# The last tile of each sequence leaves out its state update in an fp32 linear-attention and two-FFN kernel

## The reference

```
state = zeros(B, H, D, D)
for t in range(S):                       # B=4, H=8, S=768, D=48
    kt, vt, rt = k[:, :, t], v[:, :, t], r[:, :, t]
    cur = einsum('bhd,bhe->bhde', u[None] * kt, vt)
    y[:, :, t] = einsum('bhd,bhde->bhe', rt, state + cur)
    state = w[None, :, :, None] * state + einsum('bhd,bhe->bhde', kt, vt)
```

## Time and profile before

| | us |
|---|---|
| Median of 3 executions | 806.8 |
| The three executions | 805.24, 806.8, 806.94 |
| The profiled execution, its own time | 806.01 |
| Its span, from the first to the last instruction | 804.3 |
| PE busy in the span | 739.9 (92%) |
| DVE busy | 425.6 (53%) |
| ACT busy | 304.3 (38%) |
| POOL busy | 149.6 (19%) |

### The profile page before, as it was taken

The page is one execution under the profiler, slowest core; times in us unless marked ns, Lnnn a source line. Parts: engine busy times, 40 slices in busy tenths (PEclk is TensorE's granted clock), DMA queues, the critical chain, the costliest instruction groups (busy, mean ns, idle before and its releaser), DMA issues. The chain is left out here.

```text
span 804.3 us, 12788 instructions
## 1 busy us (share of the span) xinstructions
PE 739.9 (92%) x4978; PEld 619.3 (77%) x4979; DVE 425.6 (53%) x677; ACT 304.3 (38%) x505; POOL 149.6 (19%) x170
## 2 busy tenths in 40 slices
PE   3789898999999999999999999999359999999995
PEld 2668687788877887788878888888249999998985
DVE  6778765575647565475746564544354323223232
ACT  2546443543445343544444443644233212122120
POOL 7433531222222211122222200000060000000000
PEclk9999988999999999999999999999769999999998
DMA  8792110211121111111110000000360202202021
GB/s 150 197 226 48 20 30 11 70 30 21 30 69 31 31 30 22 59 30 31 28 43 1 1 1 30 11 1 1 106 212 1 79 0 79 79 1 78 0 78 39
DMA packets 88316, 40.36 MB, mean 50 GB/s; under 512 B 77112, under 2 KB 84928, under 8 KB 88256
## 3 DMA queue, kind: packets, MB, share of 16 engines
q1 hardware_dynamic: 86800, 34.61, 17.2%
q10 hardware_dynamic: 1456, 4.93, 1.6%
HBM read 30.10 MB, written 9.44 MB: 49 GB/s over the span
## 5 line engine op out<-in xcount | busy, mean ns | idle before, releaser
L856 PE MATMUL x_ps<-g_p,wout_hi 128*128 128x512 f32 x576 | 186.7, 405 | 3.5 <-DVE g_p L672 3.4
L870 PE MATMUL h_ps<-x0T,win_hi 128*128 128x512 f32 x576 | 180.1, 394 | 1.2 <-DVE x0T L601 1.2
L472 ACT ACTIVATE above<-h_ps,minus_one 128x512 f32<-128x512 f32 x96 | 65.9, 687 | 196.4 <-DVE mid L681 196.4
L681 DVE TENSOR_SCALAR mid<-h_ps 128x512 f32<-128x512 f32 x96 | 66.2, 690 | 124.7 <-PE h_ps L870 124.5
L856 PEld LDWEIGHTS x_ps<-g_p,wout_hi 128*128 128x128 f32 x576 | 104.4, 190 | 32.3 <-DVE g_p L672 6.5
L870 PEld LDWEIGHTS h_ps<-x0T,win_hi 128*128 128x128 f32 x576 | 107.5, 189 | 24.4 <-DVE x0T L601 1.5
L1401 PE MATMUL ch_ps<-x_p,w_p 128*128 128x512 f32 x432 | 109.2, 400 | 11.9 <-DVE w_p L1467 11.9
L685 DVE TENSOR_TENSOR mid<-mid,above 128x512 f32<-128x512 f32 x96 | 82.6, 861 | 70.0 <-ACT mid L473 70.0
L856 PE MATMUL x_ps<-g_p,wout_lo 128*128 128x512 f32 x288 | 113.2, 393 | 0.0
L870 PE MATMUL h_ps<-x0T,win_lo 128*128 128x512 f32 x288 | 112.6, 391 | 0.0
L1390 PE MATMUL cy_ps<-w_p,h_p 128*128 128x384 f32 x576 | 107.7, 336 | 0.0
(11 more groups left out here) (208 smaller groups left out, 652.1 us busy)
## 6 DMA issues: line engine op xcount, KB each, us to landing
xr<-xT_scratch SPq DMA_DIRECT2D x8, 768.0 KB, 4.7
rkv<-in_r SPq DMA_DIRECT2D x24, 192.0 KB, 3.0
rkv<-in_k SPq DMA_DIRECT2D x24, 192.0 KB, 3.4
rkv<-in_v SPq DMA_DIRECT2D x24, 192.0 KB, 2.8
xT_scratch<-xbuf ACTq DMA_DIRECT2D x6, 768.0 KB, 3.3
out<-acc SPq DMA_DIRECT2D x12, 384.0 KB, 2.4
win_raw<-in_moe_w_in SPq DMA_DIRECT2D x48, 64.0 KB, 2.7
wout_raw<-in_moe_w_out SPq DMA_DIRECT2D x4, 768.0 KB, 6.3
```

The costliest lines, as they stand in the source:

```text
L472: raises(act.activation(above[:, f % 2], h_ps[f % 2][:, :], ACT.Relu, bias=minus_one[:, :]), "over")
L681: raises(dve.tensor_scalar(mid[:, f % NM], h_ps[f % 2][:, :], -1.0, 1.0, ALU.max, ALU.min), "clamped")
L856: last = pe.matmul(x_ps[kk][:, :], (wout_hi, wout_lo)[a][:, f, cols], g_p[:, f % NG, b], start=(f == 0 and n == 0), stop=(f == NF1 - 1 and ...
L870: last = pe.matmul(h_ps[f % 2][:, :], (win_hi, win_lo)[a][:, f // QF, kk, cols], x0T[:, c % 2, b, kk], start=(kk == 0 and n == 0), stop=(k ...
```

## The change

For tiles 20 to 23 PE issues no `update` and DVE no `next_state`. The waits that hung on them are put elsewhere. `scale_k` waits for `u_done` of tile 19 at most, and in addition, for every tile from 4 on, for `tr_done` of the tile before. `turn_rk` waits for `stated` of tile 19 at most. `make_y` waits, in every tile, for the load of v and for both halves of `masked`, which `update` waits for as well; where there is no `update` these are the only such waits.

```diff
+        LAST = NTILE - B
...
                 def scale_k(it):
                     a = tile_set(it)
                     if it >= B:
-                        wait(dve, "u_done", it - 1)
+                        wait(dve, "u_done", min(it, LAST) - 1)
+                        wait(dve, "tr_done", it - 1)
...
                         if attn and f % 4 == 3:
-                            next_state(it)
+                            if it < LAST:
+                                next_state(it)
                             rows_low(it)
...
                     elif it > B:
-                        wait(pe, "stated", it - 1)
+                        wait(pe, "stated", min(it, LAST) - 1)
                         wait(pe, "x_lo", it - 1)
...
                     v, rest = rkv[:, b, 2], first_vz[it] if it < B else vz[:, it % 2]
+                    v_here(pe, it)
+                    wait(pe, "masked", it)
                     y = a.banks[1]
...
                             if f % 4 == 2:
-                                update(it)
+                                if it < LAST:
+                                    update(it)
                                 make_y(it)
```

## The result

| | before | changed |
|---|---|---|
| Median | 805.24 us (5 executions) | 801.44 us (5 executions) |
| Lowest and highest | 803.9 and 806.94 | 799.4 and 801.85 |
| Profiled execution, own time | 806.01 | 801.46 |
| Its span | 804.3 | 799.7 |

The ratio is 0.9947, with a 95% interval from 0.9928 to 0.9967. Measured again later, beside 11 executions of the kernel before, it was 0.9959 (0.9944 to 0.9973). The change makes the kernel faster by about half a percent.

What follows compares the result with a forecast made beforehand. PE was taken to set the pace. Part 1's 3.62 us, with parts 2 and 3 at 0, gave 802.4 from 806.01 and 803.2 from 806.8; the middle, 802.8 us, was forecast, range 801.3 to 805.1.

Steps and rivals of the forecast that it cites:

- Part 1: PE's updates in tiles 20 to 23 go: gain 3.62 us, with bounds 3.89 and 2.27.
- The 0.69 us kept for an issue limit in tile 20: Loss if y's 56 matmuls took 0.042 us each once no update precedes them; taken as 0, kept for the bound.
- the dear entry of 0.54 us: Bound on the distance from h's last matmul to y's first in tiles 21 to 23; 0.32 was taken.
- Part 2: DVE's next_state in tiles 20 to 23 goes: 1.16 us a tile beside PE, costed at 0, 1.5 us cover left.
- Part 3: Added waits in make_y and scale_k, mostly already satisfied: 0; bound 0.09 us in each of 20 tiles, 1.8 us.
- I take the middle, 802.8 us: Forecast for the whole kernel, between 802.4 from the profiled execution and 803.2 from the median of three.
- the largest gain: Upper bound of the gain from removing PE's four updates: 3.89 us.
- Columns only: Rival for PE's updates: only column time returns, 0.34 us a tile, 1.37 in all; time 805.0, chance 0.04.
- Waits at 0.09: Rival for the added waits: 0.09 us a tile, gain 1.8 us, time 804.6; chance 0.05.
- at 0.31 us: Slower rival: doubled waits in make_y hold PE 0.31 us in each of 20 tiles, 6.2 us; 809.0, chance 0.04.
- A wait in place of the work: Rival: PE waits instead, likely at the transposes behind ks in tiles 21 to 23; 805.4, chance 0.04.
- The change does nothing: Rival: the eight rows per tile of the update stay in place in tiles 20 to 23; chance 0.01.

Runs made afterwards that it cites:

- the narrow: Kernel before, but in tiles 20 to 23 the update computes only 16 of each 96 columns: 804.92 us (one execution), distance 96.49 us.
- the double update: Kernel before, but tiles 20 to 23 make the same update twice: 817.13 against 805.01 us, ratio 1.015.
- the waits alone: Kernel before with only the three added waits (v and masked ahead of y, tr_done ahead of scale_k), nothing removed: ratio 1.0007.

## Why the prediction was right or wrong

**Direction and mechanism: right.** PE's updates were on the path, and only they.

**Part 1, right in size.** 3.62 us were forecast and the distance shrank by 3.69. Tile 20 gave 1.08 (1.03 forecast), tile 21 gave (444.92 - 442.07) - (442.55 - 440.57) = 0.87 (0.86). Tile 20's 0.05 more is y's quicker start behind the mask, 0.10 us in place of 0.15. The starts of `down` in tile 21 are these, before and after:

```profile
444.92 0.73 PE L856 MATMUL x_ps<-g_p,wout_hi 128*128 128x512 f32 x2
```

```profile
442.55 0.72 PE L862 MATMUL x_ps<-g_p,wout_hi 128*128 128x512 f32 x2
```

The 0.69 us kept for an issue limit in tile 20 were not needed: y took 1.67 us without an update ahead of it. Nor was the dear entry of 0.54 us.

**Part 2, right.** 0 was forecast; leaving it out alone gave 0.04 us, putting it back cost 0.03. The cover of 1.5 us named there is 1.60 in the trace. What the prediction did not see is that ACT's copy of y takes the freed place, so DVE's x_lo comes no sooner at all.

**Part 3, right.** 0 was forecast for the waits and two runs bear it out. The 0.09 us a tile of its upper bound don't come from the two waits: the update followed h at 0.23 us behind the same two. They are likely the change of shape, since the scores stand at 0.32 behind a single wait and y at 0.31 in the changed kernel; y has two more waits of its own there, in both kernels, and no run separates those.

**The level and the lower end of the range: wrong.** This is the step "I take the middle, 802.8 us", together with "I hold the spread of the executions to be of this kind and add none for it". The middle of the profiled execution and of the median of three put the kernel before at 806.4; five executions put it at 805.24, and 31 later ones at 804.84. From 805.24 the same sum gives 805.24 - 3.62 = 801.6, and 801.44 was measured. The range's lower end, 801.3, was the lowest of three executions less the largest gain. Two of the changed kernel's five executions lie below it, and so does the ratio times the median before, 0.9947 x 805.24 = 801.0. Three executions don't show how low the next can come: the fourth and fifth took 805.03 and 803.9 us, and the 31 later ones lie between 802.67 and 807.25, 4.6 us apart where the three were 1.7 apart. So the term that the prediction put at nothing, the spread, was larger than the whole change, and the range's lower end stood too high for want of it. On which side of 801.3 a measurement then falls is partly luck: measured again, the changed kernel took 802.15. The forecast difference of 4.0 us to the median then shown was 3.62 from the sum and the rest from choosing the level; measured were 4.3 by the first ratio and 3.3 by the second.

**The rivals.** Columns only: refuted by the narrow and the double update. Waits at 0.09 and at 0.31 us: refuted by the waits alone. A wait in place of the work: no new wait on `ks` at the transposes; at tile 21 `ks` ends at 430.23 and the weight load starts at 430.28 in the changed kernel, the same margin of 0.05 us as before. The change does nothing: 32 instructions are gone.

**The pages.** The gap between matmuls in the Trainium skill's "TensorE: Matmul & The Clock Gate", section "Back-to-back issue gap", 42.5 ns for 96 columns, is not what an update costs here: 0.11 to 0.12 us an instruction, and nearly the same with 16 columns. The prediction took too little from that section: it calls this formula the gap of an isolated matmul, which "under-counts" where few columns stand beside a weight load, and gives some 81 ns, measured at 128 columns, for a stream of such pairs. The update lies above that figure too. A semaphore read of 50 to 100 ns, in "Advanced Engine Details and Errata", section "Network/Comms", adds nothing to a PE that has other work under way.

## What to carry to other kernels

Price a removed instruction by the distance between the starts of its neighbours on the engine that sets the pace, and add what the new neighbours cost each other. Small matmuls that each load 128 columns of weights are paid by the pair, 0.11 to 0.12 us here, hardly by the column. Measure a small edit by a distance between two waits that both kernels share; the total time carries clock and collisions that the edit doesn't own, and these can be larger than it.

## What was not expected of the hardware

**POOL's memset holds certain DVE instructions until it ends.** Scalar operations over 24 elements per partition lasted 7.40 and 7.44 us instead of 0.2, both ending within 0.05 us of the 7.77 us memset; a product of two tensors beside the same memset took 0.18. A reduction ran in its usual 0.35 us inside the memset of the double update (592.46), just ahead of the instruction that was held. Products of 768 elements per partition, from 591.10 on in the kernel before, run inside it too. The Trainium skill, "SBUF — State Buffer", section "Who interferes with whom", says that `tensor_scalar` can take a pair of ports which DVE shares with GpSimd, for a whole instruction, and that the loser waits fully, while a DVE instruction with two inputs only meets a GpSimd instruction that reads. By that rule, the traces agree in both. They also show its other side, which has nothing to do with the memset: in the kernel before, a product of two tensors of 64 elements on DVE lasts 1.32 us from 582.26, where its neighbour took 0.21, and ends within 0.1 us of a POOL instruction that reads two tensors (582.23 + 1.27 = 583.50):

```profile
582.01 0.21 DVE L1448 TENSOR_TENSOR grid<-grid,active 1x64 f32<-1x64 f32 x1
582.26 1.32 DVE L1449 TENSOR_TENSOR grid<-grid,number 1x64 f32<-1x64 f32 x1
```

In the kernel before, the distance to the collision with the memset is some 1.1 us, so a small shift can cost it 7 us. What made DVE late in the double update is left open: PE's counting product came at 583.52, 1.2 us after its input, which the profile gives as issue, and I did not test whether the longer program is the cause.

**A long stall can cost more than its own length.** In chunk 0, two stalls of about 3.6 us were followed by matmuls at half pace (1.90 and 1.99 us for eight that take 1.10); covering them took 8.5 us off the chunk, while the stalls themselves shrank by 5.1. That the clock accounts for the rest is read from the rows and was not tried by itself, and the third stall shows that the time at half pace behind stalls of one length differs from trace to trace, here some 7 against 3 us.
